# Rotated q/k loads fetched whole and first, weight loads put last, in a fused attention and two-layer feed-forward kernel

## The reference

```python
def rotate(x):                       # half = D // 2, cos and sin by position
    x1, x2 = x[..., :half], x[..., half:]
    return np.concatenate([x1*cos - x2*sin, x1*sin + x2*cos], axis=-1)
q_rot, k_rot = rotate(q), rotate(k)  # B, H, S, D = 4, 8, 576, 64
scores = (1/np.sqrt(D)) * q_rot @ k_rot.transpose(0, 1, 3, 2)
scores = scores - scores.max(-1)
attn = np.exp(scores); attn = attn / (attn.sum(-1) + 1e-9)
x = (attn @ v) as (2304, 512)        # tokens by heads
h = x @ w_in1;  x = (h - tanh(h)) @ w_out1     # d_ff = 2048
h = x @ w_in2;  out = (h * sigmoid(h)) @ w_out2
```

## Time and profile before

| | |
|---|---|
| median of three runs | 1088.74 us (1087.91 to 1090.46) |
| the profiled execution | 1090.46 us |
| its span, first to last instruction | 1088.7 us |
| PE busy | 1028.4 us, 94% |
| POOL busy | 718.0 us, 66% |
| DVE, ACT busy | 641.2 us, 526.7 us |
| share of PE in the chain that ended last | 78% |
| packets of the SP queue | 68528, 93.43 MB |
| raw from q and k | 30 transfers of 576 KB and 4 of 288 KB |

### The profile page before, as it was taken

One profiled execution on the slowest core, in us unless ns is written; L12 is line 12 of the kernel. 1 busy time (PEld: TensorE's weight loads), 2 busy tenths in 40 slices (PEclk: granted clock), 3 DMA queues, 4 the chain that ended last, 5 costly groups with the idle time before them and its releaser, 6 DMA issues.

```text
span 1088.7 us, 17872 instructions
## 1 busy us (share of the span) xinstructions
PE 1028.4 (94%) x7116; PEld 934.9 (86%) x7116; DVE 641.2 (59%) x887; ACT 526.7 (48%) x791; POOL 718.0 (66%) x495
## 2 busy tenths in 40 slices
PE   3999999999899999999899998999989999899998
PEld 2889999998699889998899988989878888788887
DVE  6567677765554675546754467554675555844544
ACT  2567777778343345433444335443354442544432
POOL 6798999982766665666666575665756657466550
PEclk9999999999999998999999999999999999999999
DMA  5545655532122121221212212122121421113201
GB/s 181 167 135 160 191 164 168 186 108 56 47 78 77 40 78 39 78 78 40 77 40 78 78 43 74 39 79 78 44 72 40 136 78 61 56 42 134 78 20 58
DMA packets 68610, 94.56 MB, mean 87 GB/s; under 512 B 17328, under 2 KB 44208, under 8 KB 68528
## 3 DMA queue, kind: packets, MB, share of 16 engines
q1 hardware_dynamic: 68528, 93.43, 27.0%
HBM read 84.02 MB, written 4.79 MB: 82 GB/s over the span
## 4 chain that ended last, share of the span: by engine, by line
PE 78%; DVE 9%; issue 5%; POOL 3%; ACT 2%; DMA 2%; SPq 0%; DVEq 0%; ACTq 0%; POOLq 0%
PE ps L838 29%; PE ps L877 17%; PE ps L858 16%; PE ps L703 5%; PE ps L667 4%; PE ps L697 3%; DVE xsum L1153 2%; PE ps L605 2%; DVE x_l L1157 2%; PE ps L669 1%; PE ps L657 1%; DVE hid L1205 1%; PE ps L733 1%; DVE hm L1089 1%; POOL x_l L538 1%
## 5 line engine op out<-in xcount | busy, mean ns | idle before, releaser
L534 POOL TENSOR_TENSOR win_l<-win_s,win_h 128x512 fp32r<-128x512 f32 x96 | 121.0, 1278 | 276.8 <-ACT win_h L961 276.8
L838 PE MATMUL ps<-x_h,win_l 128*128 128x384 f32 x672 | 231.1, 344 | 30.9 <-DVE hid L1205 13.6
L1021 ACT ACTIVATE th<-hid 128x768 f32<-128x768 f32 x96 | 80.5, 839 | 352.0 <-DVE hid L1205 352.0
L838 PE MATMUL ps<-x_l,win_h 128*128 128x384 f32 x672 | 229.8, 342 | 0.0
L838 PE MATMUL ps<-x_h,win_h 128*128 128x384 f32 x672 | 228.9, 341 | 0.0
L1205 DVE TENSOR_TENSOR hid<-ps,snap 128x384 f32<-128x384 f32 x192 | 106.4, 554 | 144.7 <-PE ps L838 144.7
L838 PEld LDWEIGHTS ps<-x_h,win_l 128*128 128x128 f32 x672 | 128.7, 192 | 49.1 <-DVE hid L1205 15.5
L1205 DVE TENSOR_TENSOR snap<-ps,snap 128x384 f32<-128x384 f32 x144 | 79.6, 553 | 122.0 <-PE ps L838 121.5
L1089 DVE TENSOR_REDUCE hm<-ps 128x2 f32<-128x576 f32 x144 | 108.4, 756 | 61.0 <-PE ps L605 52.6
L838 PEld LDWEIGHTS ps<-x_l,win_h 128*128 128x128 f32 x672 | 128.7, 191 | 10.2
L858 PE MATMUL ps<-g_l,wout_h 128*128 128x512 f32 (+1 forms) x384 | 132.6, 345 | 0.0
(11 more groups left out here) (100 smaller groups left out, 2141.2 us busy)
## 6 DMA issues: line engine op xcount, KB each, us to landing
win_s<-w_in SPq DMA_DIRECT2D x45, 512.0 KB, 5.0
wout_s<-w_out SPq DMA_DIRECT2D x45, 512.0 KB, 4.0
raw<-qk SPq DMA_DIRECT2D x30, 576.0 KB, 4.5
v<-vfull SPq DMA_DIRECT2D x16, 384.0 KB, 4.5
R<-inverse_sums SPq DMA_DIRECT2D x32, 144.0 KB, 3.1
vr<-vin SPq DMA_DIRECT2D x16, 192.0 KB, 3.3
out<-ostage SPq DMA_DIRECT2D x2, 1536.0 KB, 8.7
ev<-ev SPq DMA_DIRECT2D x16, 144.0 KB, 4.9
```

Source lines behind the costliest of these rows:

```text
L534: nc.gpsimd.tensor_tensor(lo, src, hi.bitcast(F32), ALU.subtract).then_inc(s_wl, 1)
L838: last = mm(ps[:, up_bank(g, i), 0:TH], a[w][:, BLOCKS[i], kk, :], b[i][:, kk, :], start=(k == 0), stop=(k == 5))
L1021: nc.scalar.activation(th[:, f, :], hid[g % 2][:, f, :], ACT.Tanh, scale=(1.0, 0.5)[g // (NT * NJ)]).then_inc(s_t, 1)
```

## The change

The two transfers of a pair's q and k become one of 1152 KB with one semaphore, so POOL waits once, before `rope_scale`'s first operation, for all four slots. In each iteration this load moves ahead of `load_split_v`, and `load_weights` moves from before `join_heads` to the end of the iteration, after `spread_inverse`. Pair 0 keeps its four separate loads. No arithmetic changes.

```diff
             def load(n):
                 sp.wait_ge(s_lq, n - 1)
-                sp.dma_start(raw[n % 2][:, 0:2, :], qk[n, :, 0:2, :]).then_inc(s_ld[n % 2], 16)
-
-            def load_swapped(n):
-                sp.wait_ge(s_lq, n - 1)
-                sp.dma_start(raw[n % 2][:, 2:4, :], qk[n, :, 2:4, :]).then_inc(s_ls[n % 2], 16)
+                sp.dma_start(raw[n % 2][:, :, :], qk[n, :, :, :]).then_inc(s_ld[n % 2], 16)
...
-            sp.dma_start(raw[1][:, 0:2, :], qk[1, :, 0:2, :]).then_inc(s_ld[1], 16)
-            sp.dma_start(raw[1][:, 2:4, :], qk[1, :, 2:4, :]).then_inc(s_ls[1], 16)
+            sp.dma_start(raw[1][:, :, :], qk[1, :, :, :]).then_inc(s_ld[1], 16)
...
             load(2)
-            load_swapped(2)
...
             for n in range(PAIRS):
+                if n + 3 < PAIRS:
+                    load(n + 3)
                 if n + 1 < PAIRS:
                     load_split_v(n + 1)
-                if n + 3 < PAIRS:
-                    load(n + 3)
                 if n >= 1:
                     gather_sums(n - 1)
-                if n + 3 < PAIRS:
-                    load_swapped(n + 3)
                 if 1 <= n < PAIRS - 1:
                     load_full_v(n + 1)
-                if n in W_LOAD:
-                    load_weights(*W_LOAD[n])
                 if n >= 1:
                     join_heads(n - 1)
...
                 if n >= 1:
                     spread_inverse(n - 1)
+                if n in W_LOAD:
+                    load_weights(*W_LOAD[n])
...
                 pool.wait_ge(s_ld[n % 2], 16 * (n // 2 + (n % 2)))
                 nc.gpsimd.tensor_tensor(t[:, 0:2, :], t[:, 0:2, :], ctab...)
-                pool.wait_ge(s_ls[n % 2], 16 * (n // 2 + (n % 2)))
                 nc.gpsimd.tensor_tensor(t[:, 2:4, :], t[:, 2:4, :], stab...)
```

More of the change, by code:

```diff
@@ L135, in attention_and_two_ffn @@
         s_ld = [sem(f"qk_loaded{i}") for i in range(2)]
-        s_ls = [sem(f"swapped_qk_loaded{i}") for i in range(2)]
         s_vr = sem("split_v_loaded")
```

## The result

The changed kernel takes 1101.27 us in the median of three runs (1098.56 to 1105.45) against 1088.74: ratio 1.0114, 95% interval 1.0073 to 1.0157. It is 12.5 us slower where 2.1 were forecast, and outside the range. The profiled execution took 1097.01 us with a span of 1095.2, the quickest of its executions, 6.5 us of span over before. Its attention stage lost more than that: the last sums are stored at 288.24 us instead of 279.43, 8.8 us later. What follows explains these 8.8 us closely, what the slower executions lost beyond them only in kind.

What follows compares the result with a forecast made beforehand. It took PE to set a period of 14.7 us a pair from 116.7 to 228.5 us. To the median 1088.74 it added 0.8 (start) and 1.3 (late v load): 1090.8 us, range for 8 in 10 1088.3 to 1094.0.

Steps and rivals of the forecast that it cites:

- the v load behind it: Steady attention iterations: v load behind weights and whole raw load lands late, holding ACT's `v_high`; +1.3 us, bounds nothing to 7.
- The cover: Between ACT's `v_high` and PE's scores of unit 7: some 0.7 us of each wait is hidden, the rest reaches PE.
- the reduction: Added bytes partly fill queue gaps (258 against 381 GB/s): 0.4 us less per landing, sum 0.7 instead of 2.2 us.
- The landing: 852 thousand bytes more at 381 GB/s land 2.2 us later; v load 1.2 us after ACT wants it in iteration 7.
- late `vr` in full: Rival: ACT waits from iteration 3 to 12 with only 0.2 us covered, 4.8 us in iterations 6 to 12; 1094.3 us, chance 0.2.
- the signs that the prediction names: Changed profile: v loads land in 5 to 7 us; ACT idles 0.5 to 1.5 us before `v_high` in iterations 7, 10, 11.
- its sign of being wrong on the side of the cost: Attention loop: PE's period growing over 14.9 us in most iterations would show the forecast cost wrong.
- The start: Pairs 1 and 2: whole loads land later, POOL rotates later, ACT's `qk_high(2)` delays pair 1's scores; +0.8 us, bounds 0.2 to 2.4.
- The merged load later on: Later iterations: whole load needed at POOL's first product, there in time with about 1 us of cover; nothing.
- The weights: Weight loads moved to the iteration's end are used one iteration later or more, so nothing waits; nothing, at best 0.5 us gained.
- Ring order or not: DMA queue: ring order makes `vr` land behind the load; rival, transfers interleave and `vr` is free, 1089.5 us, chance 0.12.
- The range: Whole kernel, 8 in 10: 1088.3, inside the hidden case, to 1094.0 us, near the late `vr` case.

Runs made afterwards that it cites:

- half dose: Against the kernel before: weights last, first half of the raw load ahead of the v load, second half at its old place; 1090.57 us, 1.0011 over before.
- merge_ahead_of_v: Changed kernel with the weight loads back at their old place, merged load still ahead of the v load; 1096.08 us, 1.0071 over the kernel before.
- halves_ahead_weights_last: Changed kernel's order without its merge: weights last, two half loads with two semaphores, then the v load; 1098.49 us, 1.0101 over the kernel before.

## Why the prediction was wrong, step by step

**The mechanism of the forecast was the right one, its size was not.** The step that failed is "the v load behind it", the term of +1.3 us. It was made of waits worked out one by one, a cover and a reduction. The cover and the reduction were both too large, and the waits were taken as separate where each one brings on the next.

- *The landing.* I let 852 thousand bytes more delay it by 2.2 us at 381 GB/s, and then took 0.4 us off each. Waits of 1.2, 0.6, 1.2, 1.6 and 1.0 us in iterations 7, 8, 10, 11 and 12 and 0.4 in 6 were the sum before that: 6.0 us. Measured are 1.64 (6), 0.48 (7), 1.06 (8), none (9), 1.25 (10), 1.38 (11), 3.58 (12): 9.4 us, and 1.01 and 0.90 in iterations 1 and 2, which I had under 0.5. Without iteration 12 the unreduced sum was near, 5.0 against 5.8. The reduction by the queue's unused share was an argument, not a measurement.
- *The cover.* I covered 0.7 us of each wait. What came through can be read by how far the next `qk_high` stood behind its old time, before and after each wait: 1.28 us of 1.64, 0.12 of 0.48, 0.68 of 1.06, 0.90 of 1.25, 1.22 of 1.38. So 0.16 to 0.38 us were covered, and of the wait of 3.58 nothing: 4.4 us came through. The way from `v_high` to the stored sums shows the same: 5.15 us before (146.71 to 151.86), 4.68 in iterations 6 to 11 wherever ACT had waited, so that it held 0.47 us of slack and no more. I had read the cover from gaps that each stood alone. Over iterations 6 to 12 the profile has 8.6 us come through where the term said 1.3.
- *The lap.* I worked out each wait against the old times of everything before it, and so missed why the waits return: a late `v_high` makes the next stored sums late, and these hold back the next v load. The lap is, in parts: store to the issue of the v load 4.2 us (154.31 to 158.47), landing 6.5 (median of iterations 6 to 12), and from `v_high` to the next store 4.7. That is 15.4 us, over PE's 14.7, and the measured period is 15.36. Once it is longer, the lap is the period, and PE does not win time back between pairs. With the half dose it is 4.5 + 4.7 + 4.7 = 13.9, under the period, and the cost nearly vanishes. In `merge_ahead_of_v`, from the store at 141.30, it is 3.98 + 7.50 + 4.67 = 16.15, and the next store comes at 157.45. By these parts the v load may take some 5.8 us to land before it costs anything in the loop, an estimate (14.7 less 4.2 and 4.7). The forecast's "late `vr` in full", 1094.3 us at a chance of 0.2, came nearest and was still too low: it used the same old times, and its sum leaves out the 0.5 us that it names for the iterations before 6.
- *The spread of times.* The timed runs reach 1105.45 us while the profiled one has 1097.01. A wait of 3.5 us or more cost 4.4 to 4.8 us with the clock's answer, and the profile of `halves_ahead_weights_last` (1103.4 us of span) has two of them. That more such landings make the slower runs is the likely reading; no profile of a run of 1105 us was taken.

Of the signs that the prediction names, those of its mechanism came: `vr` landed in 6.4 us, and ACT waited 0.48, 1.25 and 1.38 us in iterations 7, 10 and 11. So did its sign of being wrong on the side of the cost: the period was over 14.9 us in five of the seven iterations 6 to 12.

**The other steps.**

- *The start, +0.8 us.* POOL's first rotation was forecast at about 11.8 and began at 11.80; the second at 30.0 and began at 29.36: `qk_low(0)` ended at 22.26, not 22.7, and the load was issued at 23.66, not 24.1. In the profiled execution `qk_high(2)` then stood only 0.2 us behind and the scores of pair 1 began at 42.11, not 42.7; over all profiles the start costs some 1.0 us, as shown above. The size was right.
- *The merged load later on, nothing.* Right for the changed kernel but for one wait of 0.9 us in iteration 12, which lies beside the long wait of ACT. With the v load first it is not nothing: seven waits.
- *The weights, nothing.* Right by themselves (0.9999). In the changed kernel their issue is a link of the lap, 0.6 us in the chain above (157.37 to 158.00); that it adds as much to the time is not shown.
- *Ring order or not.* The v load did not overtake: `vr` landed 3.2 us after its issue where it stood first, 4.7 behind 832 KB and 6.4 behind 1408 KB. The rule of the Trainium skill's page "DMA: Bandwidth & Descriptors", section "Queues, rings and completion order", that each engine takes descriptors in ring order, agrees. By the fit of the same page of the Trainium skill, section "Anatomy of one DMA", which it gives for transfers issued from GpSimd, the v load behind 1408 KB and with its own 192 KB would take 2.0 + 1638 / 436 = 5.8 us, an estimate. The measured median is 6.4, and here SP issues them.
- *The range.* Its upper end, 1094.0, came from a case in which the same landings had less cover. It did not ask what happens when SP's issues and a landing are both slow in one lap, as in iteration 12.
- *The end.* Of the 8.8 us that the attention stage had lost the feed-forward layers give 2.3 back in this pair of profiles. Up to 370 us the changed kernel stands 8.8 us late; then the clock differs in stretches of the same work, before first:

```profile
380.00:400.00 20.00, 20.00 (x107) 18.64 (x106) 13.94 (x17) 10.39 (x14) 10.98 (x9) 0.91 0.16 54
```

```profile
388.80:408.80 20.00, 20.00 (x116) 18.66 (x115) 15.48 (x19) 10.39 (x14) 12.57 (x9) 1.00 0.17 54
```

Behind it the changed kernel is 7.3 us late, and further on between 5.1 and 8.6, where no instruction differs. What is gained there belongs to the two executions and not to the change.

## What to carry to other kernels

When a small transfer that someone waits for is put behind a large one, work out the lap that the wait closes, from its own release back to itself, and compare it with the period of the engine that sets the pace: under it the cost was nearly nothing here, over it the whole excess was paid each time. Count in it the time in which SP issues the transfers, and take each part where its wait binds: read from the kernel before, a part still holds slack. A merge of transfers, and an order of issues, are two edits and need two prices; here the merge cost 0.26% (0.14 to 0.38) and the order 0.8 to 1%. If the order must stay, moving the consumer (here `v_high`, by 6 us) gives that second part back.

## What the runs showed of the hardware

- A transfer of 192 KB landed after 3.2, 4.7 and 6.4 us (medians) with nothing, 832 KB and 1408 KB issued just before it, and after 6.8 with 1152 KB in another kernel (`merge_ahead_of_v`). The last does not fit a sum of bytes.
- PE's granted clock fell behind each of its three long gaps in the loop: with 2.82 us before 231.58 it averaged 0.57 from 230 to 238 us, with 2.74 and 2.86 us in `halves_ahead_weights_last` 0.79 over the 8 us after. Gaps of 0.49 to 0.89 us in iterations 6 to 11 of the changed kernel, and one of 1.35 in the other, left it at 1.00.
- Single issues of SP took 1.3 us and more in place of 0.4 to 0.7 now and then (1.30 for a copy and 1.37 for a spread before the long landing of iteration 12; up to 1.40 and 1.69 in the kernel before). On SP they lie in the lap like any other work.
